# Gated linear attention and a two-layer mixer in fp32: scores of two batches from keys and queries split in device memory

## The reference

```
m_new = max(f + m, i);  C = exp(f + m - m_new) * C + exp(i - m_new) * outer(v, k)
n = exp(f + m - m_new) * n + exp(i - m_new) * k
y = sigmoid(o) * (C q) / max(|n q|, 1)
x = y as [batch, 768, 320]
u = x + transpose(relu(transpose(x) w_tok1) w_tok2)
out = u + relu(u w_ch1) w_ch2
```

## Time and profile before

| | |
|---|---|
| median of three runs | 456.74 us (455.03 to 456.75) |
| the profiled execution, its own time | 456.15 us |
| its span | 454.4 us |
| TensorE busy | 438.0 us (96%), 3463 products |
| VectorE, ScalarE, GpSimd busy | 259.2 (57%), 208.4 (46%), 209.4 (46%) us |
| DMA | 47.38 MB, mean 104 GB/s |

### The profile page before, as it was taken

How to read it: one execution, slowest core, us unless ns; L and a number is a source line. 1 busy time by engine, 2 the same in 40 slices (tenths; PEclk the granted TensorE clock), 3 DMA queues, 4 the chain that set the end, 5 groups by cost and what they waited for, 6 DMA issues and landing times.

```text
span 454.4 us, 9503 instructions
## 1 busy us (share of the span) xinstructions
PE 438.0 (96%) x3463; PEld 407.1 (90%) x3463; DVE 259.2 (57%) x592; ACT 208.4 (46%) x517; POOL 209.4 (46%) x293
## 2 busy tenths in 40 slices
PE   7899989998999999899999999899999999999996
PEld 3587889898999988799999998899999998999996
DVE  8689874788875346777664137677664326213122
ACT  3766368655554248655552137655652213211120
POOL 7624421788896333888861204798883000000000
PEclk9999999999999999999999999999999999999999
DMA  7667990442344415434444013434410010000101
GB/s 211 205 203 215 334 249 10 123 144 96 100 130 145 126 43 170 123 107 134 124 151 142 1 44 104 147 119 142 126 61 1 1 43 1 0 2 0 45 1 43
DMA packets 36616, 47.38 MB, mean 104 GB/s; under 512 B 3356, under 2 KB 29082, under 8 KB 36570
## 3 DMA queue, kind: packets, MB, share of 16 engines
q1 hardware_dynamic: 35674, 45.76, 33.4%
q10 hardware_dynamic: 896, 1.02, 0.6%
HBM read 42.73 MB, written 4.03 MB: 103 GB/s over the span
## 4 chain that ended last, share of the span: by engine, by line
PE 77%; ACT 6%; issue 6%; DVE 5%; DMA 4%; POOL 1%; ACTq 0%; DVEq 0%; POOLq 0%
PE pC L1156 30%; PE pA L1227 6%; PE pA L1228 6%; PE pA L1229 6%; PE pS L1068 6%; PE pA L1156 5%; DMA x<-o_gate_dram 4%; PE pY L1125 4%; PE pA L1231 3%; PE pA L1232 3%; PE pY L1104 2%; PE pN L1080 2%; DVE gb L856 1%; DVE pb L865 1%; ACT h_hi L760 1%
## 5 line engine op out<-in xcount | busy, mean ns | idle before, releaser
L979 DVE SCALAR_TENSOR_TENSOR h_lo<-pA,h_hi 128x384 fp32r<-128x384 f32 x96 | 53.4, 557 | 146.4 <-ACT h_hi L760 146.4
L760 ACT ACTIVATE h_hi<-pA 128x384 fp32r<-128x384 f32 x96 | 46.7, 487 | 135.2 <-PE pA L1232 135.2
L1156 PE MATMUL pC<-wc_hi,h_hi 128*128 128x320 f32 x288 | 94.1, 327 | 1.0 <-DVE wc_lo L846 0.9
L1156 PE MATMUL pC<-wc_lo,h_hi 128*128 128x320 f32 x288 | 88.7, 308 | 0.0
L1156 PE MATMUL pC<-wc_hi,h_lo 128*128 128x320 f32 x288 | 88.4, 307 | 0.0
L494 POOL TENSOR_TENSOR gb<-gb,pb 128x384 f32<-128x384 f32 (+1 forms) x54 | 51.7, 958 | 65.4 <-ACT pb L628 65.1
L1227 PE MATMUL pA<-uT_hi,wc_hi 128*128 128x384 f32 x192 | 65.2, 340 | 0.2 <-DVE wc_lo L846 0.2
L1228 PE MATMUL pA<-uT_lo,wc_hi 128*128 128x384 f32 x192 | 64.7, 337 | 0.0
L1229 PE MATMUL pA<-uT_hi,wc_lo 128*128 128x384 f32 x192 | 64.3, 335 | 0.0
L1156 PEld LDWEIGHTS pC<-wc_hi,h_hi 128*128 128x128 f32 x288 | 54.0, 188 | 2.3 <-DVE h_lo L979 1.2
L1156 PEld LDWEIGHTS pC<-wc_lo,h_hi 128*128 128x128 f32 x288 | 54.2, 188 | 0.1
(11 more groups left out here) (135 smaller groups left out, 879.9 us busy)
## 6 DMA issues: line engine op xcount, KB each, us to landing
gb<-g_dram SPq DMA_DIRECT2D x18, 512.0 KB, 4.0
kv<-kvN_dram SPq DMA_DIRECT2D x24, 324.0 KB, 3.7
kd<-kT_dram SPq DMA_DIRECT2D x24, 180.0 KB
qz<-qT_dram SPq DMA_DIRECT2D x72, 60.0 KB
out_dram<-u SPq DMA_DIRECT2D x24, 160.0 KB, 1.9
qd<-qT_dram SPq DMA_DIRECT2D x20, 180.0 KB, 2.5
gq<-g_dram SPq DMA_DIRECT2D x45, 60.0 KB
wc_raw<-w_ch_dram SPq DMA_DIRECT2D x6, 384.0 KB, 5.6
```

What stands on the lines that cost most here:

```text
L760: nc.scalar.activation(h2[0][:, slot % 2], pA[slot % 2][:, 0:HALF], ACT.Relu).then_inc(h2_hi, 1)
L979: nc.vector.scalar_tensor_tensor(h2[1][:, slot % 2], pA[slot % 2][:, 0:HALF], 0.0, h2[0][:, slot % 2].bitcast(F32), ALU.max, ALU.subtract) ...
L1156: ins = mm(dst, a[p], b[q], start=first and n == 0, stop=last and n == 2)
```

## The change

Keys and queries of batches 2 and 3 come a second time as one input qk, per chunk 120 rows (three groups of 40) of 2 x 384 values. While the attention of batches 1 and 2 runs, each chunk of the next batch is loaded (load_raw), split by ScalarE (a copy to fp32r, the high part) and VectorE (the difference, the low part), and both parts are stored to a tensor `halves` in device memory. For a step, three loads of 40 rows put [key high, query low], [key low, query high] and [key high, query high] on top of each other into one of four places of `stack`, and the score of each head is one fp32r product over 120 rows, 128 by 128. Batches 0 and 1 keep kd, qz and the fp32 products. The exponential of gq moves from chunk_start to one step later, behind v_middle; gq has two buffers instead of three after batch 0. SyncE's order is changed accordingly. Some early constants now share memory with later buffers.

```diff
+HALVED = 2
+RING = 4
+HALVES_AT = 5
...
+        halves = nc.dram_tensor("halves", [B - HALVED, NC, ROWS, 4, GH * L], F32, kind="Internal").ap()
...
+        stack = sb("stack", [ROWS, RING, 2, GH * L])
...
+        qk_raw = sb("qk_raw", [ROWS, 2, GH * L])
+        qk_high = sb("qk_high", [ROWS, 2, GH * L], F32R)
...
-        gq = sb("gq", [ROWS, Q, NG, L])
+        gq = sb("gq", [ROWS, R, NG, L])
...
+        def halved(ba, m):
+
+            i, rest = divmod(m - HALVES_AT, NG)
+            return NC * (ba + 1 - HALVED) + i if rest == 0 and 0 <= i < NC and HALVED <= ba + 1 < B else None
...
+            def load_raw(n):
+
+                if n > 0:
+                    sp.wait_ge(halves_out, 16 * HALVES_DMAS * n)
+                sp.dma_start(qk_raw[:, :, :], qk[n // NC, n % NC]).then_inc(raw_in, 16)
+
+            def store_halves(n):
+                row = halves[n // NC, n % NC]
+                sp.wait_ge(halved_hi, n + 1)
+                sp.dma_start(row[:, 3, :], qk_high[:, 0, :].bitcast(F32)).then_inc(halves_out, 16)
+                sp.dma_start(row[:, 0, :], qk_high[:, 1, :].bitcast(F32)).then_inc(halves_out, 16)
+                sp.wait_ge(halved_lo, n + 1)
+                sp.dma_start(row[:, 1:3, :], qk_raw[:, :, :]).then_inc(halves_out, 16)
+
+            def load_step(ba, m):
+
+
+                c, g = divmod(m, NG)
+                k = stacked(ba, m)
+                sp.wait_ge(halves_out, 16 * HALVES_DMAS * (NC * (ba - HALVED) + c + 1))
+                sp.wait_ge(s_mm, STEPS * HALVED + max(k - RING + 1, 0))
+                rows_g = halves[ba - HALVED, c, g * D:(g + 1) * D]
+                for i, pair in enumerate((slice(0, 2), slice(2, 4), slice(0, 4, 3))):
+                    sp.dma_start(stack[i * D:(i + 1) * D, k % RING], rows_g[:, pair, :]).then_inc(stack_in[k % RING], 16)
...
+            def load_chunk(ba, c):
+
+                halving = ba + 1 if HALVED <= ba + 1 < B and c >= R else None
+                first = NC * (ba + 1 - HALVED)
+                load_decays(ba, c)
+                if halving and c > R:
+                    store_halves(first + c - R - 1)
+                if ba < HALVED:
+                    load_scores(ba, c)
+                else:
+                    load_step(ba, NG * c)
+                    load_step(ba, NG * c + 1)
                 load_values(ba, c)
                 if c > 0:
-                    load_inter(ba, c)
-
-            def load_chunk(ba, c):
-                load_scores(ba, c)
-                load_rest(ba, c)
+                    load_query_decays(ba, c)
+                if halving:
+                    load_raw(first + c - R)
+                if ba >= HALVED:
+                    load_step(ba, NG * c + 2)
+                if c > 0:
+                    load_queries(ba, c)
...
+            def next_batch(ba):
+
+                first = NC * (ba - HALVED)
+                load_decays(ba, 0)
+                store_halves(first + 3)
+                load_values(ba, 0)
+                load_raw(first + 4)
+                store(ba - 2, 0)
+                load_decays(ba, 1)
+                store_halves(first + 4)
+                load_raw(first + 5)
+                for m in range(RING):
+                    load_step(ba, m)
+                load_values(ba, 1)
+                load_query_decays(ba, 1)
+                load_queries(ba, 1)
+                store_halves(first + 5)
+                store(ba - 2, 1)
+                for m in range(RING, 2 * NG):
+                    load_step(ba, m)
...
             def chunk_start(ba, c):
                 n = NC * ba + c
                 fill = ba * (NC // R) + c // R + 1
-                if c > 0:
-                    act.wait_ge(gq_in[c % Q], 16 * GQ_DMAS * gq_fills(ba, c))
-                    nc.scalar.activation(gq[:, c % Q], gq[:, c % Q], ACT.Exp).then_inc(gq_exp, 1)
...
                 if ba > 0 and m % NG == 0 and 0 <= m < STEPS:
                     v_middle(ba, m // NG)
+                    if m > 0:
+                        query_decays(ba, m // NG)
+                n = halved(ba, m)
+                if n is not None:
+                    act.wait_ge(raw_in, 16 * (n + 1))
+                    nc.scalar.activation(qk_high[:, :, :], qk_raw[:, :, :], ACT.Copy).then_inc(halved_hi, 1)
...
+                n = halved(ba, m)
+                if n is not None:
+                    dve.wait_ge(halved_hi, n + 1)
+                    nc.vector.tensor_tensor(qk_raw[:, :, :].bitcast(F32R), qk_raw[:, :, :], qk_high[:, :, :].bitcast(F32),
+                                            ALU.subtract).then_inc(halved_lo, 1)
...
+                if ba >= HALVED:
+                    i = stacked(ba, m)
+                    pe.wait_ge(stack_in[i % RING], 16 * STACK_DMAS * (i // RING + 1))
+                    keys_i, queries_i = [stack[:, i % RING, side, :].bitcast(F32R) for side in range(2)]
+                    for j in range(n):
+                        cols = slice(j * L, (j + 1) * L)
+                        last = mm(scores_bank(ba, m)[:, cols], keys_i[:, cols], queries_i[:, cols], start=True, stop=True)
+                    last.then_inc(s_mm, 1)
+                    return
```

More of the change, by code:

```diff
@@ L79, in step_in, with program @@
     return slot - BEHIND if b == 0 else slot + AHEAD
-def program(nc, qT, kT, kvN, i_gate, f_gate, o_gate, w_tok1, w_tok2, w_ch1, w_ch2, out):
+def program(nc, qT, kT, qk, kvN, i_gate, f_gate, o_gate, w_tok1, w_tok2, w_ch1, w_ch2, out):
     ctx = ExitStack()
@@ L109, in program, with first @@
         qd = sb("qd", [ROWS, R, NG, L])
-        kd = sb("kd", [ROWS, R, NG, L])
-        qz = sb("qz", [ROWS, R, NG, GH, L])
+        with ExitStack() as early:
+            kd = early.enter_context(nc.sbuf_tensor("kd", [ROWS, R, NG, L], F32))
+            qz = early.enter_context(nc.sbuf_tensor("qz", [ROWS, R, NG, GH, L], F32))
+        stack = sb("stack", [ROWS, RING, 2, GH * L])
+        with ExitStack() as early:
+            def first(name, shape, dt=F32):
+                return early.enter_context(nc.sbuf_tensor(name, shape, dt))
+            gp = first("gp", [3 * NH, S], BF16)
+            g_mid = first("g_mid", [NH, S], BF16)
+            eye = first("eye", [128, 128], BF16)
+            above = first("above", [128, L], BF16)
+            pick = first("pick", [3 * NH, NH], BF16)
+            pick_q = first("pick_q", [3 * NH, NG * GH, D], BF16)
+            gq_first = first("gq_first", [ROWS, NG, L])
+        qk_raw = sb("qk_raw", [ROWS, 2, GH * L])
+        qk_high = sb("qk_high", [ROWS, 2, GH * L], F32R)
         kv = sb("kv", [128, R, KV])
@@ L163, in program, with gq_at @@
         pN = bank("pN")
+        def gq_at(ba, c):
+            if ba == 0:
+                return gq_first[:, :, :] if c % Q == R else gq[:, c % Q]
+            return gq[:, c % R]
         def scores_bank(ba, m):
@@ L184, in program @@
         gb_in = [sem(f"gb_in{i}") for i in range(Q)]
-        gq_in = [sem(f"gq_in{i}") for i in range(Q)]
+        gq_in = [sem(f"gq_in{i}") for i in range(R)]
+        raw_in = sem("raw_in")
+        halved_hi = sem("halved_hi")
+        halved_lo = sem("halved_lo")
+        halves_out = sem("halves_out")
+        stack_in = [sem(f"stack_in{i}") for i in range(RING)]
         g_out = sem("g_out")
@@ L295, in gq_fills, with stacked @@
         def gq_fills(ba, c):
-            return (ba - 1) * (1 if c % Q == 0 else 2) + (1 if c <= Q else 2)
+            return (ba - 1) * (NC // R - (1 if c % R == 0 else 0)) + (c + 1) // R
+        def stacked(ba, m):
+            return STEPS * (ba - HALVED) + m
+        def halved(ba, m):
+            i, rest = divmod(m - HALVES_AT, NG)
+            return NC * (ba + 1 - HALVED) + i if rest == 0 and 0 <= i < NC and HALVED <= ba + 1 < B else None
         def segment(c):
@@ L305, in program @@
         GQ_DMAS = 3
+        HALVES_DMAS = 3
+        STACK_DMAS = 3
         @block.sync
@@ L421, in _ @@
                 if b < B - 2:
-                    load_scores(b + 2, 0)
-                store(b, 0)
-                if b < B - 2:
-                    load_rest(b + 2, 0)
-                    load_chunk(b + 2, 1)
-                store(b, 1)
+                    next_batch(b + 2)
+                else:
+                    store(b, 0)
+                    store(b, 1)
             for half in range(2):
@@ L886, in state @@
                 nc.vector.tensor_tensor(stn[0:n * D, 0:n, :], sums, keep, ALU.mult).then_inc(n_read, 1)
[L888 removed]
+                fade = gq_at(ba, c)[0:n * D, g, L - 1:L]
                 dve.wait_ge(gq_exp, inters(ba, c))
@@ L1062, in step_scores @@
                 n, r = HEADS[g], c % R
-                if g == 0:
+                if g == 0 and ba < HALVED:
                     pe.wait_ge(qk_in[r], 16 * QK_DMAS * (ba * (NC // R) + c // R + 1))
@@ L1270, in rows, with by_step @@
         return np.ascontiguousarray(padded.reshape(B, NG, ROWS, NC, L).transpose(0, 3, 2, 1, 4))
+    def by_step(a):
```

(4 more changed lines are left out.)

55 lines of the change are left out of this document (29 added, 26 removed).

## The result

The changed kernel takes **467.24 us** (median of four runs, 466.32 to 467.57) against 456.43 (455.03 to 456.75) for the kernel before on the same chips: a ratio of 1.0234, with a 95% interval of 1.0201 to 1.0266. It is 2.3% slower, where 449.6 and "faster" had been forecast, and it lies outside the range. The span of the profiled execution is 464.6 us, 10.2 longer than that of before.

The account below looks back on a forecast made before the run. TensorE was taken to bound the slots, and a chain through ScalarE and VectorE the border. Per batch 5.7-0.95-0.51 = 4.2, for two 8.5, less 1.9 for transfers: 6.6 off 456.15, giving 449.6 us; range 446.5 to 460.0.

Parts of the forecast that it names:

- What the change takes off TensorE: Score steps of batches 2 and 3: 0.098 us per head in fp32r, gaining 0.95 us per chunk, 5.7 per batch.
- rival 1: Scores: fp32r of 128 columns runs at the fp32 rate, 0.229 us per head, 458.4 us in all; chance 0.28.
- rival 2: Smaller gain: load and stream in sequence, 0.164 per head (453.0), or batch 1 loses its chunks' gain (451.5); chance 0.15.
- (a) Splitting hidden in batch 0: ScalarE copy and VectorE subtraction per chunk, 12 times: taken as 0 in batch 0's slots; uncovered, 1.9 us a chunk.
- (b) SyncE's queue: Issues of 7 to 8 of 11.6 us per chunk: not full; kv holds by one or two us, raw data without margin.
- (c) Bytes: Ten engines need 11.8 to 14.2 us per batch 1 chunk; loss between 0 and 10.4 us, taken as 1.9.
- Rival 3: Slower by transfers: full engines and SyncE waiting make batch 1's chunks 14 to 16 us, 458.5 to about 465.7; chance 0.12.
- What is lost at the border: Between batches: 0.95 us of saved scores doesn't count and the moved exponential adds 0.51, leaving 4.2 net per batch.
- steps 2 to 4: Score steps falling between 173 and 189 us at the border, whose savings of 0.95 us were said not to count.
- No clock effect is in play: Whole profile before the change: granted clock 1.00 (2.4 GHz) in every slice, so no clock loss was priced.
- The signs to look for: Score times, slot gaps, batch 1 waits with DMA share above 0.8, border gap about 1.4 us longer, batch 0 within 1 us.

Follow-up runs that it names:

- combo: Changed kernel with kv_act's orders, step loads 4 and 5 behind o_gate, second chunk's gq exponential back ahead of the gate; batch 2 102.0 us, whole no faster than before.
- no_split: Changed kernel without splitting batch 3 in batch 1's slots, its scores reading batch 2's halves (wrong values); 0.2% faster than the kernel before, batch 1 104.7 us.
- kv_soon: Changed kernel with the raw load behind the first step load and, in batch 1, kv's load ahead of the halves' stores; ratio 1.0132 to the kernel before.
- before_2: The kernel before, unchanged, run once more to see whether the start's time spreads by itself; start above 51 us.
- gq_late: Kernel before with only the gq exponential a step later, batches 1 to 3; costs 1.1 us in batch 1 and 2.3 in batch 2 against before_again.
- before_again: The kernel before, unchanged, run once beside kv_soon and other experiments; batches 1 and 2 are compared with it.
- one_combo: combo with HALVED = 3, so only batch 3 is split; 454.41 us, 0.5% less than the kernel before (0.2 to 0.7).
- one_batch: Changed kernel with only batch 3's keys and queries split and only its scores fp32r; batch 1 109.3 us, batch 2 104.4 us.
- kv_act: kv_soon with ScalarE's copy of the split behind the high of x; batch 1 110.4 us, as a whole not told from kv_soon.
- raw_soon: Changed kernel with the next raw load right after the first step load in batch 1's slots; ratio not told from the changed kernel's, batch 1 115.3 us.

## Why the prediction was wrong

The prediction had batch 1 gain 2.3 us (4.2 less 1.9) and batch 2 gain 4.2, and the rest unchanged. By the means of the table batch 1 lost 7.5, batch 2 gained 0.4, batch 0 lost 1.7, and start and end 1.1 together. Of the 16.4 us between the two, 9.8 stand in batch 1, 3.8 in batch 2, 1.7 in batch 0.

- **What the change takes off TensorE**: right. 0.28 us per three heads for 0.29; rival 1 (the fp32 rate) and rival 2's 0.49 fall. The slots of batch 2 give 0.85 of the 0.95 us a chunk.
- **(a) Splitting hidden in batch 0**: nearly. Its price was right (837 ns for the copy, 958 for the subtraction, by the rows of 832 and 1031), but batch 0's chunks take 12.9 us instead of 12.55, and the batch lost 1.7 us, 0.9 of it from slot 4 on. With ScalarE's copy behind the high of x (combo) its chunks are at 12.6 again, and from slot 4 on it takes 80.2 us (80.4 before, 81.3 in the changed kernel): the order on ScalarE was that part of the price, which "hidden" left out. The other 0.8 is the spread until slot 4 (27.5 to 29.7 us in the changed kernel, 27.6 to 28.2 before).
- **(b) SyncE's queue**: the right place, and then no price. The text said that the raw data "has no margin", that stores wait for the halves and the next raw load for the stores; but it didn't add up the ring. From rows that it had: raw data landing with the 3.7 us median of kv, 0.83 and 1.03 for the engines, and the issues of a store, two steps, kv and the query decays, eleven of 0.34 to 0.76, 4 to 5: about 10 us at the median landing, under 11.6, and 15 to 16 at the 9.3 us that the same rows have as the longest. So the rows said that it hung on the landing under load, and the text took it at the median ("lands by 201"). What happened was 7.54 + 0.85 + 0.97 and 5.3 of issuing, 14.7. kv of chunk 3 left at 202.16, 198.5 on the clock of before (batch 1 began 3.6 later) and not near 197, and took 6.72 us to land and not 3.7: 205.3 where its reader had been forecast for 203.4. SyncE's issues were counted about right (7.4 and 8.2 us in two rounds, of 7 to 8), and a queue that is half empty was the bound all the same.
- **(c) Bytes**: "I take half of what those chunks gain, 1.9", is the step that failed worst. The bounds were 0 and 10.4 us of loss over four chunks; the stores of the stalled stretch leave every 14.0 us, and from slot 4 on the batch takes 7.7 us more than without the ring (no_split). So the size lay within the bounds, and the half that was taken had no row behind it. The throughput of the ten engines was the wrong measure: kv_soon moved the same bytes at 12.95, and the raw data landed in 3.5 to 4.2 us or in 6.2 to 7.5 at the same DMA share, by their place in the order. Rival 3 named the chunk (14 to 16 us) and the sign; at 14.4 us a chunk its sum gives 459.3, 3 of the 11 us measured. Its batch 1 comes out at +7.4 for 7.5, in part by luck: 2.8 of the 7.5 stand before slot 4, and it kept the 4.2 of batch 2. Its chance of 0.12 was too small, because it was argued from throughput, where the ring of waits needed no full engine.
- **What is lost at the border**: right in its terms, wrong as a sum. The 0.51 us of the exponential stands on the chain, and the 0.95 of steps 2 to 4 vanish. Not priced were the gate's transfer behind the step loads (5.05 us for 3.50 at batch 2's border), and that a longer gap can be followed by half the clock: up to 3.4, 5.1 and 3.4 us in the batches of the three executions. Batch 2's border (first mixing product to slot 4) takes 35.14 us instead of 33.36, 1.8 more where 0.2 less had been summed, and eats two thirds of the 2.84 us that its fourteen following slots gain. "No clock effect is in play" was read from before, and held only for the gaps of before. In combo, with the gate first and one exponential back, the batch gains 3.4 to 3.8 us: that supports these terms together; their shares were not separated.
- **The signs to look for**: "I am wrong if ... the border, not the slots, takes the time" was one of two causes; the other was the waits in batch 1, with the DMA share above 0.8 named there. "Batch 0 unchanged within 1 us" missed by 0.7.

Left open: the last slots of each batch take 2.73 us in every kernel made from the changed one and 2.71 in before, before_2 and gq_late, 0.3 us over batch 3. It is not the program alone: in before_again they take 2.71 until slot 13 of batch 3 and 2.73 from slot 14 on. Nothing here says why. What beside a gap brings the half clock isn't settled either.

## What to carry to other kernels

Where an edit adds a producer to an in-order queue, add up the ring of waits round which one buffer goes (landing, engines, landing, the issues in between), at the landing times of the loaded queue and at its place in the order, and compare it with the pace you hope for: a queue or DMA share well under one says nothing about it. A microsecond taken off the bounding engine counts only where it stays the bound; ask what the stage before and after it does with it, and keep work that moved off one place from standing at the border of two stages. Move each part of such a change to where it fits (here one batch instead of two, one exponential in the old place, the others in the new) before judging it as a whole.

## What the hardware showed that was not expected

TensorE's half clock (1.2 instead of 2.4 GHz) stood behind gaps of 1.60 us (kv_soon), 1.66 (one_combo), 1.75 (gq_late), 2.13 (one_batch) and 2.42 (the changed kernel, batch 1); but the gap of 2.42 at the next border was not followed by it, nor were 2.25 and 2.42 in kv_act's batch 1, 1.66 in combo's batch 2, and 1.24 in the kernel before, whose gaps from batch 0 on are 1.28 at most. The gap alone does not decide it: the same gap of 2.42 us at batch 2's border was followed by the half clock in one of three executions of the changed kernel. In the batches it always came in or behind a gap, never within gapless slots; once there it can last: in one_combo's trace TensorE counts as busy for 24.00 of 24.00 us from 41 to 65, at a granted clock of 0.51. The same transfer of raw data took from 3.7 to 7.5 us to land in the changed kernel, and 3.5 to 4.2 where only its place in SyncE's order was another (raw_soon).
